# Attention and expert layers on one core: the value products of the second query half as one burst

## What is computed

```python
B, H, S, D = 4, 8, 576, 64
scores = scale * q @ k.T + bias[head]          # (B, H, S, S)
attn = exp(scores - max) / (sum + 1e-9)
attn_out = attn @ v                            # (B, H, S, D)
```

## Time and profile before

| | us |
|---|---|
| median of 3 runs | 1845.45 (1844.3 to 1845.69) |
| the profiled execution | 1844.29 |
| its span, first to last instruction | 1842.5 |
| PE busy | 1826.9 (99%) |
| PE weight loads busy | 1590.0 (86%) |
| DVE busy | 1054.5 (57%) |
| POOL busy | 1028.1 (56%) |
| ACT busy | 824.6 (45%) |
| PE's share of the chain that ended last | 95% |

### The profile page before, as it was taken

The page is one execution under the profiler, slowest core; times in us unless marked ns, Lnnn a source line. Parts: engine busy times, 40 slices in busy tenths (PEclk is TensorE's granted clock), DMA queues, the critical chain, the costliest instruction groups (busy, mean ns, idle before and its releaser), DMA issues.

```text
span 1842.5 us, 27892 instructions
## 1 busy us (share of the span) xinstructions
PE 1826.9 (99%) x10223; PEld 1590.0 (86%) x10223; DVE 1054.5 (57%) x1784; ACT 824.6 (45%) x1416; POOL 1028.1 (56%) x720
## 2 busy tenths in 40 slices
PE   8999999999999999999999999999999999999999
PEld 4677777798999999999999999999999999999998
DVE  8877777778554555456545554555465545544553
ACT  8877777533433333344333333333333333333331
POOL 0223326577666666666776666666666666666661
PEclk9999999999999999999999999999999999999999
DMA  7764562021111111112121122121121111111210
GB/s 229 243 150 97 129 148 68 23 92 53 65 67 69 69 69 69 69 69 103 69 69 69 69 69 69 69 69 69 70 103 69 69 69 69 69 69 69 69 46 35
DMA packets 44127, 152.47 MB, mean 83 GB/s; under 512 B 9584, under 2 KB 18032, under 8 KB 29680
## 3 DMA queue, kind: packets, MB, share of 16 engines
q1 hardware_dynamic: 44016, 150.99, 25.5%
HBM read 135.63 MB, written 15.34 MB: 82 GB/s over the span
## 4 chain that ended last, share of the span: by engine, by line
PE 95%; DVE 1%; ACT 0%; POOL 0%; issue 0%; POOLq 0%; DVEq 0%
PE banks L660 14%; PE banks L661 14%; PE banks L659 14%; PE banks L627 13%; PE banks L631 13%; PE banks L629 13%; PE banks L557 4%; PE banks L518 3%; PE banks L500 3%; PE banks L501 2%; PE banks L571 1%; PE banks L528 0%; PE banks L678 0%; ACT probs L786 0%; DVE x_lo_rest_r L1081 0%
## 5 line engine op out<-in xcount | busy, mean ns | idle before, releaser
L1279 POOL TENSOR_TENSOR w_lo<-stage,w_hi 128x1024 fp32r<-128x1024 f32 (+1 forms) x288 | 647.4, 2264 | 525.7 <-ACT w_hi L832 524.7
L1161 DVE TENSOR_TENSOR u<-p_copy,banks 128x384 f32<-128x384 f32 x192 | 106.3, 554 | 632.0 <-PE banks L631 632.0
L661 PE MATMUL banks<-w_hi,h_lo 128*128 128x512 f32 x1152 | 450.1, 391 | 0.0
L660 PE MATMUL banks<-w_lo,h_hi 128*128 128x512 f32 x1152 | 449.9, 391 | 0.0
L659 PE MATMUL banks<-w_hi,h_hi 128*128 128x512 f32 x1152 | 449.0, 390 | 0.0
L1167 DVE SCALAR_TENSOR_TENSOR h_lo<-corner,h_hi 128x384 fp32r<-128x384 f32 x384 | 412.7, 1102 | 0.0
L879 ACT ACTIVATE h_hi<-corner 128x384 fp32r<-128x384 f32 x384 | 196.5, 526 | 270.9 <-DVE corner L1161 267.9
L627 PE MATMUL banks<-x_hi,w_hi 128*128 128x384 f32 x896 | 300.6, 335 | 0.0
L631 PE MATMUL banks<-x_hi,w_lo 128*128 128x384 f32 x896 | 300.2, 335 | 0.0
L832 ACT ACTIVATE w_hi<-stage 128x1024 fp32r<-128x1024 f32 (+1 forms) x288 | 271.6, 974 | 8.8 <-POOL stage L1273 8.8
L868 ACT ACTIVATE p_copy<-banks 128x384 f32<-128x384 f32 x96 | 47.4, 493 | 491.0 <-PE banks L631 491.0
(11 more groups left out here) (130 smaller groups left out, 2472.2 us busy)
## 6 DMA issues: line engine op xcount, KB each, us to landing
stage<-in_expert_w SPq DMA_DIRECT2D x96, 1024.0 KB, 4.8
raw<-in_qk SPq DMA_DIRECT2D x32, 576.0 KB, 7.2
bias_scratch<-bias_out SPq DMA_DIRECT2D x36, 288.0 KB, 2.6
bias<-bias_scratch SPq DMA_DIRECT2D x16, 288.0 KB, 2.9
v_main<-in_v SPq DMA_DIRECT2D x16, 256.0 KB, 2.7
bias<-bias_scratch SPq DMA_DIRECT2D x16, 256.0 KB, 3.8
out<-total SPq DMA_DIRECT2D x4, 768.0 KB, 4.0
out<-total SPq DMA_DIRECT2D x6, 256.0 KB, 2.0
```

The lines of the kernel that those rows point to most:

```text
L660: pe.matmul(dst, h_hi[:, g % 2, f, tokens], lo[:, f], start=False, stop=False)
L661: mm = pe.matmul(dst, h_lo[:, g % 2, f, tokens], hi[:, f], start=False, stop=fp == FPAIRS - 1 and f == 1)
L1161: dve.tensor_tensor(out, other, bank, op).then_inc(combined, 1)
L1279: pool.tensor_tensor(lo, of, hi.bitcast(F32), ALU.subtract).then_inc(w_split, 1)
```

## The change

The three entries of half 1 become one, at the place of the first of them: step 1 of the next batch, behind `turn`, all five chunks of keys. The steps in which DVE copies the halves out are now given by a table of their own, `HEADS_AT`: half 0 as before in step 0 of the next batch, half 1 in step 2 instead of step 3. `columns_free`, `values` and the wait of ACT's first `round_weights` read the number of parts from the tables and follow.

```diff
-PV_PARTS = ((4, 0, range(0, 3), False), (5, 0, range(3, 5), True),
-            (6, 1, range(0, 2), False), (7, 1, range(2, 3), False), (8, 1, range(3, 5), True))
-PV_DONE = (2, 5)
+PV_PARTS = ((4, 0, range(0, 3), False), (5, 0, range(3, 5), True), (6, 1, range(0, 5), False))
+PV_DONE = (2, 3)
+HEADS_AT = (5, 7)
...
                 for half in range(2):
-                    after = PV_PARTS[PV_DONE[half] - 1][0]
-                    if (s - after) % QC == 0 and exists(hp, s - after):
-                        keep_heads(hp, s - after, half)
+                    if (s - HEADS_AT[half]) % QC == 0 and exists(hp, s - HEADS_AT[half]):
+                        keep_heads(hp, s - HEADS_AT[half], half)
```

## The result

| | before | changed |
|---|---|---|
| median, us | 1844.88 (1844.3 to 1845.69, 4 runs) | 1862.57 (1861.67 to 1864.56, 4 runs) |
| profiled execution: span, us | 1842.5 | 1861.4 |

The changed kernel is slower: ratio 1.0099, 95% interval 1.0086 to 1.0111. The forecast was 1862, with the POOL chain as its cause.

What follows compares the result with a forecast made beforehand. The POOL chain, 10.52 us from step 2's scores, was to end last: 3.08 + 3.35 + 1.47 + 10.52 = 18.42 us a batch. Over 14 batches +15.8, batch 15 +0.5, tail +1.2: 1862 us, range 1851 to 1867.

Steps and rivals of the forecast that it cites:

- POOL chain: Per batch, from T over ACT's second rounding and POOL's two instructions to PE: 10.52 us, slack 0.44, ends last.
- T: Start of step 2's scores on PE; claimed 1.47 us later in each batch, by six products moved ahead.
- The ring: Copies by ACT and DVE that PE waits for in steps 2 to 4; PE ready at T + 9.83.
- The layout: Estimate of steps 2 to 4 from T with batch 10's durations, giving PE ready at T + 9.83 instead of 10.96.
- rival 2: In the batches, POOL chain not met, copies by ACT and DVE alone hold: 17.73 us a batch, 1852; chance 0.12.
- The sum: 14 batches of 18.42 us, +15.8; batch 15 +0.5; tail +1.2; 17.5 us in all, 1861.8.
- Nothing gives these times back: Experts' stage after attention: keeps PE covered, so the 15.8, 0.5 and 1.2 us lost before it stay lost.
- Rival 1: Whole of attention: PE alone sets the pace, 10.2 us come off, 1834; chance 0.05.
- rival 3: Batches: ring tighter, chain looser than laid out, PE's saving nearly pays for the burst: within 0.2%; chance 0.05.

Runs made afterwards that it cites:

- burst_round_early: Changed kernel with ACT's two roundings of the next batch moved from steps 1 and 2 to steps 0 and 1; 1850.1 us.
- burst_heads_late: Changed kernel with DVE's copy of half 1 put back in step 3, the ten products staying in step 1; 1860.59 us.
- two_groups_2_8: Changed kernel with half 1 split: chunks 0 and 1 in step 1, 2 to 4 in step 3, copy in step 3; 1841.25 us.
- two_groups_2_7: Like two_groups_2_8, but chunks 2 to 4 stand at the end of step 2 instead of in step 3; 1848.1 us.

## Why the prediction was right

**T later by 1.47 us.** Step 1 grew by 1.48 (3.35 to 4.83). The ten products took 2.58 us, as in the earlier trace rows.

**The chain from T.** Forecast 10.52, in batch 10 it was 10.50 us. Its length did not depend on the change. That it is what ends last is shown by three kinds of runs: PE's wait disappears when the rounding moves (12.5 us back), it appears when only POOL gets longer (+11.3 us), and the batch follows the number of products ahead of T (17.08 to 17.46 us for one chunk).

**The ring as the second limit.** The layout put PE's way at T + 9.83, with the transposes of step 3 at 4.0, step 4 at 4.9, its copy by ACT at 6.4 and its transposes at 7.1. The trace has 4.02 (252.66), 4.97, 6.35 (254.99) and 7.07 (255.71), and PE ready near 9.8 (the last values at 8.17, plus the 1.60 us that the layout gave them). That made rival 2 the next case and not a guess: it was the state that burst_round_early uncovered, at 17.49 us a batch, as its edit also takes the rounding from ahead of ACT's copy in step 4; the 17.73 us with the rounding in place are an estimate that no run measured. I had priced rival 2 with the copy of half 1 in step 2, and so its repair (burst_heads_late's edit) as worth nothing in the batches; under the POOL wait that is right, without that wait it is 0.19 us a batch.

**The sum.** 14 batches: 18.42 us forecast, 18.43 measured, +15.9 us (332.95 less 317.04 for the start of batch 15). Batch 15 and the tail: forecast +1.7; PE's second spread moved from 341.29 to 358.64, 17.35 us, of which 1.4 are past batch 14. Batch 15 made 0.2 of them instead of the 0.5 forecast: its ten products moved from 332.60 to 348.75, 16.15 us, against 15.91 at its start. The tail made the 1.2 us forecast. So 17.35 us stand against 17.5, and the two executions of the changed kernel whose mean granted clock was 1.000 spanned 1859.9 and 1860.1 us, 17.4 to 17.6 above 1842.5.

**What failed.** "Nothing gives these times back" was right, but it left out that they could be added to: I took the experts' stage as unchanged, and named a change of it as a sign that I was wrong. In the profiled execution it began on a lowered clock (below), and that execution's span is 1.3 to 1.5 us longer than those of the two at full clock. These two took 1861.67 and 1861.89 us, which is the sum of 1861.8. That the median came within 0.6 us of 1862 is in part luck: it depends on how many of the four executions met a lowered clock, which the forecast did not have.

**The rivals.** Rival 1 (PE alone, 1834) fell: PE's saving of 0.66 us a batch did not show in any kernel with one burst, not even with both costs removed (17.30 against 17.29). A group does have a price: two_groups_2_8 gained 0.21 us a batch with one group less. But the saving on PE counted only where the loops over the other engines left room for it. The Trainium skill (TensorEngine Tiling (Array Packing), Key Properties) says that changing the tiling mode drains TensorE. The gain agrees with that, but no run here shows that draining is what a group's price consists of. Rival 2 is answered above, and rival 3, a loss within 0.2%, fell with the ratio of 1.0099.

## What to carry to other kernels

PE at 99% busy says nothing about slack in a loop that passes through three other engines once per batch. Add that loop up from its last dependence on PE (here 10.5 of 10.96 us) before putting work ahead of that dependence: here all that was put ahead of it beyond the slack was paid in full, and what was taken away behind it gave nothing back once the loop ended last. A half-busy engine can be the one that ends last (here POOL, at 55%), and lengthening it on purpose by a known amount measures its slack.

## What was not expected of the hardware

After PE's wait of 2.35 us in the tail, with 0.30 us of PE work in 2.64 us, the granted clock was 0.52 for the next 3.45 us, which is almost all at the lower of its two levels, 1.2 GHz. The products then stood 0.32 us apart (359.53 to 359.85), where 0.17 us is usual. Four executions of the changed kernel have mean clocks of 1.000, 1.000, 0.999 and 0.998 and times of 1861.67, 1861.89, 1863.25 and 1864.56 us. In burst_round_early's profile the same wait of 2.35 us was followed by a clock of 1.00. PE's waits of 0.65 us at each batch's start were never followed by a lower one.

The tail is not the only place. The profiles of two_groups_2_8 (first pair of rows) and two_groups_2_7 (second pair) show the same fall far ahead of it, in code that is the same in the changed kernel, after PE had waited 1.58 us before attention's first product (61.55) and 2.14 us in the bias table's stage (21.64):

```profile
60.00:63.29 3.29, 1.30 (x8) 1.10 (x9) 2.24 (x5) 0.76 (x2) 0.00 (x0) 1.00 0.90 296
63.29:66.94 3.65, 3.65 (x18) 3.63 (x18) 2.83 (x7) 2.90 (x7) 0.00 (x0) 0.53 0.68 208
```

```profile
18.51:21.80 3.29, 1.15 (x10) 0.38 (x8) 3.29 (x7) 1.04 (x2) 0.00 (x0) 1.00 0.43 159
21.80:25.30 3.50, 3.50 (x31) 2.32 (x31) 2.91 (x7) 3.50 (x6) 0.00 (x0) 0.51 0.46 176
```

The changed kernel waited the same 1.58 us before its first product of attention (61.31), and its clock stayed at 1.00 there. Of 25 executions of before, whose wait in the tail is 1.00 us, 7 have a mean clock of 0.999 and times of 1845.64 to 1846.17 us, against 1844.22 to 1844.69 us for the rest. So such a fall costs some 1.4 us, and every kernel here is open to it. That the tail's wait brought it about in the changed kernel's profile is read from the order of the rows and not shown by a run; where the clock fell in the executions without a profile isn't known.
